# A windowed-attention head pipeline: each unit turned one slot later, and zero products at two fixed slots

## What is computed

```python
scores = scale * q @ k.T                    # per batch and head
keep = is_sink | in_window                  # first 4 keys, or the last 128
a = softmax(where(keep, scores, -1e9))
x = (a @ v) as (1536, 512)
x = (silu(x @ w_gate) * (x @ w_val)) @ w_out          # 512 -> 1536 -> 512
h = x @ w_in2
out = (max(h, 0) + alpha * min(h, 0)) @ w_out2        # 512 -> 2048 -> 512
```

## Time and profile before

| what | value |
|---|---|
| median of 3 runs | 634.06 us (633.85 to 634.45) |
| profiled execution: its time | 634.14 us |
| profiled execution: span of its instructions | 632.4 us |
| PE busy | 621.3 us, 98% of the span |
| POOL busy | 452.6 us, 72% |
| DVE busy | 409.6 us, 65% |
| ACT busy | 244.2 us, 39% |
| granted TensorE clock | 1.00 in the mean |

### The profile page before, as it was taken

How to read it: one execution, slowest core, us unless ns; L and a number is a source line. 1 busy time by engine, 2 the same in 40 slices (tenths; PEclk the granted TensorE clock), 3 DMA queues, 4 the chain that set the end, 5 groups by cost and what they waited for, 6 DMA issues and landing times.

```text
span 632.4 us, 9382 instructions
## 1 busy us (share of the span) xinstructions
PE 621.3 (98%) x3072; PEld 487.9 (77%) x3072; DVE 409.6 (65%) x696; ACT 244.2 (39%) x585; POOL 452.6 (72%) x600
## 2 busy tenths in 40 slices
PE   8889999999999999999999999999999999999997
PEld 4467776776777888888887888887888888888886
DVE  5855566666486966564747474898786567756474
ACT  5636554545545532121212030445534424442150
POOL 7847778787778989998989574689999887810000
PEclk9999999999999999999999999999999999999999
DMA  9343323321222001221202321100222222000004
GB/s 301 112 151 101 128 91 118 118 68 51 71 81 84 34 35 59 67 68 41 67 34 67 100 84 50 41 11 17 68 66 67 68 67 84 17 1 0 2 17 183
DMA packets 29391, 45.67 MB, mean 72 GB/s; under 512 B 2880, under 2 KB 9024, under 8 KB 29344
## 3 DMA queue, kind: packets, MB, share of 16 engines
q1 hardware_dynamic: 29200, 44.81, 21.5%
q10 hardware_dynamic: 144, 0.26, 0.1%
HBM read 41.92 MB, written 3.15 MB: 71 GB/s over the span
## 4 chain that ended last, share of the span: by engine, by line
PE 93%; POOL 2%; DVE 2%; ACT 1%; issue 1%; DMA 1%; SPq 0%; DVEq 0%; ACTq 0%; POOLq 0%
PE ffn_ps L1987 29%; PE att_ps L1962 24%; PE ffn_ps L1902 15%; PE att_ps L1987 8%; PE ffn_ps L1962 6%; PE att_ps L1849 3%; PE att_ps L1811 2%; PE att_ps L1828 2%; POOL scratch L1752 1%; PE att_ps L1902 1%; PE att_ps L1859 1%; DMA raw_weights<-pieces 1%; PE ffn_ps L1811 0%; PE att_ps L1805 0%; ACT L2031 0%
## 5 line engine op out<-in xcount | busy, mean ns | idle before, releaser
L1672 POOL TENSOR_TENSOR w_lo<-raw_weights,w_hi 128x512 fp32r<-128x512 f32 (+1 forms) x128 | 155.6, 1215 | 10.3
L1671 POOL CAST w_hi<-raw_weights 128x512 fp32r<-128x512 f32 (+1 forms) x128 | 79.9, 624 | 31.3 <-PE ffn_ps L1987 17.3
L2333 DVE TENSOR_TENSOR scratch<-ffn_ps,scratch 128x512 f32<-128x512 f32 x108 | 74.0, 687 | 34.7 <-PE ffn_ps L1987 34.2
L1700 POOL TENSOR_TENSOR w_lo<-part_sum,w_hi 128x256 fp32r<-128x256 f32 x80 | 59.7, 746 | 6.4
L1902 PE MATMUL ffn_ps<-x_hi,w_hi 128*128 128x512 f32 x152 | 61.7, 406 | 0.7 <-DVE x_lo L2242 0.6
L1902 PE MATMUL ffn_ps<-x_hi,w_lo 128*128 128x512 f32 x152 | 59.5, 391 | 0.0
L1902 PE MATMUL ffn_ps<-x_lo,w_hi 128*128 128x512 f32 x152 | 59.2, 390 | 0.0
L1752 POOL TENSOR_TENSOR scratch<-scratch,inv 128x264 f32<-128x264 f32 (+1 forms) x48 | 30.0, 626 | 31.4 <-DVE inv L2205 31.3
L1987 PE MATMUL ffn_ps<-h_hi,w_hi 128*128 128x512 f32 x130 | 51.7, 397 | 0.0
L1987 PE MATMUL ffn_ps<-h_hi,w_lo 128*128 128x512 f32 x130 | 50.7, 390 | 0.0
L1987 PE MATMUL ffn_ps<-h_lo,w_hi 128*128 128x512 f32 x130 | 50.6, 390 | 0.0
(11 more groups left out here) (210 smaller groups left out, 1577.3 us busy)
## 6 DMA issues: line engine op xcount, KB each, us to landing
raw_weights<-pieces SPq DMA_DIRECT2D x122, 256.0 KB, 2.7
k_sb<-kt SPq DMA_DIRECT2D x12, 264.0 KB, 3.5
v_sb<-vt SPq DMA_DIRECT2D x12, 256.0 KB, 2.7
out<-scratch SPq DMA_DIRECT2D x12, 256.0 KB, 2.0
q_sb<-qt SPq DMA_DIRECT2D x11, 256.0 KB, 3.9
scratch<-vs SPq DMA_DIRECT2D x1, 384.0 KB, 4.9
q_sb<-qt ACTq DMA_DIRECT2D x1, 256.0 KB, 2.5
alpha<-alpha_t SPq DMA_DIRECT2D x1, 8.0 KB, 6.3
```

Of the source, the lines that this page charges most:

```text
L1671: chain(pool.tensor_copy(hi, raw[:, r % n_raw, at]))
L1672: last = pool.tensor_tensor(lo, raw[:, r % n_raw, at], hi.bitcast(F32), ALU.subtract)
L1700: pool.tensor_tensor(lo, s, hi.bitcast(F32), ALU.subtract).then_inc(split_done, 1)
L2333: ins = dve.tensor_tensor(to, back_ps(key), total, ALU.add)
```

## The change

The head gets a slot form and a lag of its own: slot w is (w, w-1, w-3, w-4). Turn and spread of a unit lie three slots behind its scores, values four; scores, maximum, reciprocal and normalisation stay where they were. The head has 20 slots instead of 19. Every later slot's number n is one higher than before, for the same units, and with it go the parity by which POOL takes one or two jobs, and the rounds of SP's loop. The products of zeros ahead of the turns go (2, 4, 2 and 2); the 6 ahead of the scores of unit 2 stay, and 4 come ahead of the scores of unit 3.

```diff
+    HEAD_LAG = 4
+
+    def head_slot(w):
+        return ("slot", tuple(u if 0 <= u < early else None for u in (w, w - 1, w - HEAD_LAG + 1, w - HEAD_LAG)))
...
-    for w in range(early + LAG):
-        item = slot(w, 0, early)
+    for w in range(early + HEAD_LAG):
+        item = head_slot(w)
...
-    for n in range(early + LAG, len(slot_plan)):
+    for n in range(early + HEAD_LAG, len(slot_plan)):
         for _ in range(1 if n % 2 or plan[slot_plan[n] + 1][0] == "tsum" else 2):
...
-                if n_slot < early + LAG:
+                if n_slot < early + HEAD_LAG:
                     if n_slot in (1, 2, early, early + 1):
...
-            fills = {0: 2, 1: 4, 2: 2, early - 2: 2}
+            fills = {2: 6, 3: 4}
...
-                if u in fills:
-                    keep_busy(fills[u], bank(home(u, early), 2))
                 pe.wait_ge(norm_done, u + 1)
...
-                    if n[0] == 2:
-                        keep_busy(6, bank(att_ps, 2))
+                    if n[0] in fills:
+                        keep_busy(fills[n[0]], bank(att_ps, 2))
```

## The result

| | before | after |
|---|---|---|
| median | 634.25 us (633.85 to 635.25, 6 runs) | 649.78 us (646.50 to 653.05, 6 runs) |
| ratio | | 1.0238, 95% interval 1.0203 to 1.0273 |
| profiled execution | 634.14 us | 650.49 us, 16.35 us more |
| its granted clock, mean | 1.000 | 0.987 |

The changed kernel is 2.4% slower. Lines after L872 have moved by 4 to 6: the scores are L1809, L1811 with L1813, and L1817, `values` is L1853, `turn` L1832, the split L1677 and L1678, `normalise` L1758, a piece's issue L1589, the first feed-forward product L1906.

What follows compares the result with a forecast made beforehand. PE's own work was taken to bound the kernel from 41.6 us on, so head savings and new PE waits count one for one: 634.1 - 2.5 (head) + 12.8 (four stalls) = 644.4 us, range 637 to 650.

Steps and rivals of the forecast that it cites:

- Direction and cause: Behind the head: slower, chance 0.85, because moved slot numbers put pieces behind keys and POOL's jobs block normalisations.
- the rivals of 646 to 650 us: Clock falls after stalls or in the head, 646 to 650 us, chance 0.13; head gains nothing, 647 us, chance 0.05.
- The four stalls: PE waits for late normalisations at the turns of units 18, 22, 26 and 34: 12.8 us together, bounds 7.6 to 16.4.
- landing taken: Landing time assumed for the late piece in a stall's price: 4.5, 3.4 and 4.2 us; unit 34 not costed from its rows.
- The head: Later turn in the head ends PE's waits for POOL: gain 2.5 us, bounds 3.65 gained or 1.0 lost.
- The last normalisation: At the head's end: starts 3.1 us earlier, the DVE bound of 3.65 us less 0.5 us.
- The drain: At the head's end: DVE has one more spread, about 0.69 us, of which 0.6 us shows as loss.
- The clock: Rival: clock falls after the stalls or in the head, one to four times, 646 to 650 us, chance 0.13.
- Its sign: Products showing longer durations behind a stall would point to the rival of a falling clock.
- the six slow zero products: First six took 2.93 us, six later ones 1.66; so a slow stretch of 3 us loses 1.3 to 1.5 us.
- The zeros: Products of zeros moved in the head lie in PE's waits for POOL or ACT: nothing by themselves.

Runs made afterwards that it cites:

- e1: Changed kernel with both the parity of POOL's jobs and SP's rounds for keys and values set back by one: 631.44 us, ratio 0.9960.
- e2: Changed kernel with only SP's rounds for keys and values set back by one, POOL's parity left moved: 631.47 us, ratio 0.9962.
- e4: Kernel before with one empty slot added at the end of its head, its lag and zeros kept: 654.06 us, ratio 1.0308.
- e5: Changed kernel with ten useless products ahead of PE's wait in the turns of units 18, 22, 26 and 34: 644.40 us, ratio 1.0167.
- e6: Kernel before with only the products of zeros moved to their new places, lag and slot numbers kept: 634.50 us, ratio 1.0004.
- e7: e1 with the products of zeros in the places of the kernel before: 632.29 us, ratio 0.9965.
- e10: e8 without the ten products of zeros ahead of the scores of units 2 and 3: 635.29 us, ratio 1.0009.
- e8: Changed kernel with SP sending pieces ahead of keys from round 17 on, slot numbers and parity left moved: 631.80 us, ratio 0.9961.
- e3: Changed kernel with only the parity of POOL's jobs set back, SP's rounds left moved: 638.55 us, ratio 1.0074.
- e9: e3 with SP sending pieces ahead of values and keys from round 17 on: 631.92 us, ratio 0.9963.

## Why the prediction was right, point by point

**Direction and cause** held. e1, e2 and e4 show the cause one part at a time: numbering alone makes the loss (e4), setting SP's part of it back removes all of it (e2).

**The number** held by little. 644.4 us were forecast, with 641 to 648 for the forecast itself and 637 to 650 as the range; 649.78 were measured, past the former and 0.2 us inside the latter, and two of the six runs (650.49 and 653.05) lie above it. That the time stays inside is in part luck: the range reached that far only by the rivals of 646 to 650 us. What the sum describes, stalls and head at full clock, is nearer to e5, at 644.40 us.

**The four stalls**, from the wait to the turn that is later than it would be (from the start of the values to that of the turn, less the 0.59 us, or 0.37 us at unit 26, that this takes where nothing waits; so the sum lies 0.3 us above the 12.3 of PE's waits):

| unit | forecast | measured | landing taken | landing measured |
|---|---|---|---|---|
| 18 | 3.8 | 2.7 | 4.5 | 3.5 |
| 22 | 2.9 | 4.0 | 3.4 | 4.6 |
| 26 | 3.4 | 3.3 | 4.2 | 3.8 |
| 34 | 2.7 | 2.6 | - | 3.3 |
| sum | 12.8 | 12.6 | | |

The sum is right in part by luck: the two that are off by 1.1 us are off by their landing. The landings, taken at the same places of the kernel before, were 1.0 us too long at unit 18 and 1.2 us too short at unit 22, which cancelled.

**The head**: forecast 2.5, measured 2.1. The last normalisation starts at 34.43 instead of 36.97 (2.5 earlier, forecast 3.1). The drain takes 39.45 - 34.43 = 5.0 us instead of 4.6 (0.4 more, forecast 0.6). The errors, 0.6 us too much gained and 0.2 us too much lost, cancel in part, and the gain itself was only 1.0 and 1.4 us in the profiled runs of e2 and e5. What bounds the head now is DVE, as said: over the stretch of rows 3

```profile
11.90:36.70 24.80, 21.97 (x183) 12.63 (x183) 23.22 (x63) 15.92 (x76) 21.99 (x42) 1.00 0.55 172
```

DVE is busy 23.22 of 24.80 us instead of 21.15, and PE has no wait for POOL left in the head.

**The clock** was the term that I left out of the sum and gave as a rival with 0.13, at 646 to 650 us. It came in all six runs (0.984 to 0.995), so that this rival and the stalls hold together, and the time lies at the rival's upper end. Its sign came as named: products behind three of the stalls show 0.63 us, where they show 0.39 otherwise. The step that failed is the weighing: I had four waits of 2.7 to 3.8 us on PE in my own sum, and no row with such a wait at full clock, and still put the clock aside because the trace of before showed none falling. The price per fall was 1.6 to 2.6 us, where I had taken 1.3 to 1.5 from the six slow zero products: the slow stretches lasted 3.4 to 5.6 us instead of 3. The Trainium skill, page "TensorE: Matmul & The Clock Gate", Part 1, says that a long idle gap drops the engine to half rate until it has been busy again. The trace of the changed kernel agrees after waits of 3.92, 3.21 and 2.50 us, and shows no fall after the one of 2.66 us. With the 6.1 us that were left over above, the sum is 644.4 + 6.1 = 650.5, the profiled time, but that is no second proof: the errors of the stalls (0.5 too many) and of the head (0.4 too many) cancel in it, and the 6.7 us read from the timelines give 651.1.

**The zeros**: "nothing by themselves" held for moving them (e6, e7), and would have failed for taking them out (e10, 3.5 us above e8), which the change does not do.

**What was left out**: the values' transfers of SP's queue. In the changed kernel POOL waits 2.2 and 2.3 us for pieces behind them (issued at 70.61 and 95.94), but PE never does; in e3 PE does.

## What to carry to other kernels

A constant that counts slots, and a parity on it, tie transfers and side work to a stage's length; when a slot is added, write out every queue that counts it, in order, and look for a transfer that now stands behind one that waits. In a queue that issues in order, send what nothing holds up ahead of what waits for late work; here that one swap, with the numbering left moved, turned +15.5 us into -2.6 us (e9, with the mixed numbering of e3, had the pieces ahead of the values too). Whether a swap holds for other numberings was not tried. And where a sum holds waits of PE of 2 us and more, put the clock's fall behind them into the sum, not beside it.

## What the runs showed of the hardware

The fall of the clock is not tied to the length of one wait alone. In the profiled runs of the changed kernel, e3 and e4, the slow products followed waits of PE of 3.92, 3.64, 3.43, 3.21, 2.84, 2.50 and 2.07 us, and not waits of 2.66, 2.55 and 1.43 us. The widest pair is 2.07 us (e3), with a fall, and 2.66 us (the changed kernel's turn at 59.94, shown above), without one; the turn itself shows the pace, 0.66 us against 0.41:

```profile
93.93 0.66 PE L1832 MATMUL att_ps<-ident,scratch 128*128 128x128 f32 x2 [2.07 <-POOL scratch L1758]
```

What else enters stays open.

How the clock runs in the head differs between runs of the same kernel: nine runs of e9 took 631.5 to 632.8 us, and the profiled one 634.8, with the lower level from 13.0 us to past 20. Taking the ten useless products out (e10 against e8) made slow heads the rule, with nine of twelve runs above 634 us; by what the products act is not shown.

And a piece of 256 KB behind keys and queries in the same queue landed after 3.3 to 4.6 us in nine cases of the kernels before and after; right behind values it took 2.8 to 3.4 us in eight, and the one issued by itself 2.6 us. What makes the difference was not tested.
